# Identity matmuls ahead of the first scores, head 8's scores in other banks, and channel weights behind the v groups

## The chip, the cores and the metric

The kernel runs on one core of a Trainium2 chip. The metric is the device time of one execution in microseconds (us). Its engines are TensorE (PE in the profile, with PEld for its weight loads), VectorE (DVE), ScalarE (ACT), GpSimd (POOL) and SyncE (SP), which issues the DMA transfers. Each engine works through its own queue in order, and the queues meet in semaphores only.

## The reference

Three blocks follow each other, for a batch of 4, 8 heads, 576 positions and a head width of 64. Attention is masked by blocks of 64: query i sees key j where i // 64 >= j // 64.

```python
scores = scale * q @ k.T                      # per batch and head, masked by blocks of 64
attn = softmax(scores);  x = attn @ v         # heads side by side: x is (4, 576, 512)

h = relu(x @ w_in)                            # w_in 512 x 1024
u, v = h[..., :512], h[..., 512:]
v_n = (v - mean(v)) / sqrt(var(v) + 1e-6)
v_s = einsum('ts,bsd->btd', w_spatial, v_n) + b_spatial
y = (u * v_s) @ w_out                         # w_out 512 x 512

xn = (y - mean(y)) / sqrt(var(y) + 1e-6) * g_ln
out = y + relu(xn @ w_ch1) @ w_ch2            # w_ch1 512 x 2048, w_ch2 2048 x 512
```

## The kernel before

All of it is written out by hand, one instruction stream for each engine, with semaphores between them.

**Attention** takes 32 heads n = 0 to 31, eight to a batch. A head's queries are five tiles of up to 128 rows. Their order is 3, 0, 2, 1, 4 (`TILES`); the first three are the "first" tiles, the last two the "second" ones. For each, TensorE makes the scores in PSUM (L951) and adds a mask (L955), VectorE takes the row maximum (L759), ScalarE the exponential with its row sum (L564), VectorE inverts the sums (L767, L772), GpSimd multiplies them in (L476), TensorE transposes the result (L999), VectorE (L778) and ScalarE (L575, L576, L579) copy it out of PSUM, and TensorE multiplies by v (`attend`, L1013, L1018). The scale of q is put on by GpSimd (`scale_q`, L470). A head has four steps. On TensorE, step 0 of head n holds the first scores of head n+1, attend of head n-1 and the first transposes of head n; step 2 holds the second scores of head n+1 and the second transposes of head n.

**PSUM** has eight banks. First scores use banks 0 and 1. Second scores use two banks, given by `second_banks`: 2 and 3 for heads 0 to 7, and 1 and 2 from head 8 on, because banks 3 and 4 then belong to the mixer. With banks 1 and 2, second scores wait for the first exponentials of their own head (`score_second`), and the next head's first scores for all five (`score_first`).

**The mixer** (second block) of a batch is 26 groups of matmuls: 5 "v", 8 "u", 8 "s" and 5 "w" groups, numbered so that U0 = 5, S0 = 13 and W0 = 21. Groups of batch b are woven into the heads of batch b+1, some three to a head; the first one stands behind step 2 of head 8. They use banks 3 and 4 in turn, and each waits until the bank's last user was read (`bank_free`). A product is three FP32R matmuls of high and low parts (L1032, L1033, L1034). A v tile is copied out with a relu by ScalarE (L625), its mean and variance are made by VectorE (L812, L814, L816), the power -0.5 by GpSimd (L487), then VectorE normalises (L833), ScalarE makes the high part (L607) and VectorE the low part (L802); there are two buffers, so the copy of tile i waits for the low part of tile i-2. A u group is read by ScalarE (L629).

**The last mixer** (batch 3) has no heads beside it, and in its place the channel weights are prepared: 16 "units" of a column block of w_ch1 and a row block of w_ch2. A unit is loaded by SP, scaled with g_ln by GpSimd (`scale_unit`, L529), split in high parts by ScalarE (`split_unit`, L686, L687) and low parts by VectorE (L877, L879). `UNIT_AFTER` gives for the first ten units the group g at which GpSimd scales; ScalarE splits at g+1, VectorE at g+2, and SP then loads the unit four further on. GpSimd waits for nothing in u groups, so it runs ahead of the other engines there.

**The third block** takes six chunks of 384 rows with all 16 units (L1032 to L1034 again, L722, L925). The change leaves it as it is.

Of the kernel before, what the change touches and what calls it, by code (L numbers as in the profile page):

```python
# [27 lines left out]
P = 128  # L28
# [6 lines left out]
def transformer_block(nc, qk, vN, w_in, wsT, w_out, gT, w_ch1, w_ch2, out):  # L35
    B, H, D, S = qk.shape[0], qk.shape[1], qk.shape[2] // 2, qk.shape[3] // 2
# [5 lines left out]
    NT = -(-S // P)  # L42
# [18 lines left out]
    with ExitStack() as ctx:  # L61
        def sb(name, shape, dt=F32):
            return ctx.enter_context(nc.sbuf_tensor(name, shape, dt))

        def sem(name):
            return ctx.enter_context(nc.semaphore(name))
# [72 lines left out]
        ident = sb("ident", [P, P])  # L139
# [16 lines left out]
        psum = ctx.enter_context(nc.psum_tensor("psum", [P, 8, 512], F32))  # L156
        m_bank = psum[:, 3:5, :]
        o_bank = psum[:, 5, :]
        t_bank = psum[:, 6:8, :]
# [10 lines left out]
        ident_set = sem("ident_set")  # L170
# [3 lines left out]
        exped = sem("exped")  # L174
# [47 lines left out]
        U0, S0, W0 = NV, NV + NU, NV + NU + NS  # L222
# [3 lines left out]
        def kind_of(g):  # L226
            return ("v", g) if g < U0 else ("u", g - U0) if g < S0 else ("s", g - S0) if g < W0 else ("w", g - W0)
# [28 lines left out]
        AT = [TILES.index(t) for t in range(NT)]  # L256
        MADE = {3: 1, 0: 3, 2: 3, 1: 4, 4: 5}
        FIRST = 3

        def second_banks(n):  # L260
            return psum[:, 2:4, :] if n < H else psum[:, 1:3, :]

        def score_of(n, t):
            if t == 0:
                return psum[:, 1, KEYS[2]:KEYS[2] + KEYS[0]]
            if t == 2:
                return psum[:, 1, 0:KEYS[2]]
            if t == 3:
                return psum[:, 0, 0:KEYS[3]]
            if t == 1:  # L270
                return second_banks(n)[:, :, HALF:HALF + P]
            return second_banks(n)[0:LAST, :, 0:HALF]
# [28 lines left out]
        def bank_free(eng, b, g):  # L301

            if b == 0 and g < 2:
                if g == 0:
                    eng.wait_ge(exped, NT * H)
                return
            b, g = (b, g - 2) if g >= 2 else (b - 1, g - 2 + GROUPS)
            kind, i = kind_of(g)
            if kind == "s":
                eng.wait_ge(gate_raw, NS * b + i + 1)  # L310
            else:
                eng.wait_ge(copied, NCOPY * b + (g if g < S0 else g - NS) + 1)
# [27 lines left out]


        UNITS_EARLY = 10
        UNIT_AFTER = [1, 3, 5, S0 - 1, S0 + 1, S0 + 3, S0 + 5, W0 - 1, W0, W0 + 1]
        assert len(UNIT_AFTER) == UNITS_EARLY and UNIT_AFTER[-1] + 2 < GROUPS
        AFTER_U, AFTER_S, AFTER_W = 3, 7, 13
        assert UNITS + 2048 * AFTER_U <= MIXER and UNITS + 2048 * AFTER_S <= VN_END - 2 * NT * FFH
# [2 lines left out]
        def unit_at(g, lag):  # L349
            return [f for f, after in enumerate(UNIT_AFTER) if after + lag == g]  # L350

# [110 lines left out]
        def _(pool):  # L462
# [10 lines left out]
            def normalise(n, t):  # L473
                r, c = ROWS[t], slice(P_AT[t], P_AT[t] + KEYS[t])
                pool.wait_ge(inverted, 2 * n + (1 if AT[t] < FIRST else 2))
                pool.tensor_scalar(probs[0:r, n % 2, c], probs[0:r, n % 2, c], row_inv[0:r, n % 2, AT[t]:AT[t] + 1], 1.0,  # L476
                                   ALU.mult, ALU.mult).then_inc(normed, 1)
# [28 lines left out]
            pool.wait_ge(consts_set, 2)  # L506
            for t in TILES[:FIRST]:
                normalise(0, t)
            for n in range(HEADS):
                for step in range(STEPS):  # L510
                    if step == 0:
                        for t in TILES[FIRST:]:
                            normalise(n, t)
                        if n + 2 < HEADS:
                            scale_q(n + 2)
                    elif step == 1 and n + 1 < HEADS:
                        for t in TILES[:FIRST]:
                            normalise(n + 1, t)
# [34 lines left out]
        def _(act):  # L553
            def exp_tile(n, t):
                r, k, s = ROWS[t], KEYS[t], n % 2
                act.wait_ge(maxed, NT * n + PEAKS[t])
                if n >= 2:
                    act.wait_ge(t_made, NT * (n - 2) + AT[t] + 1)
                if n >= 2 and AT[t] == 0:
                    act.wait_ge(inverted, 2 * (n - 1))  # L560
                dst = probs[0:r, s, P_AT[t]:P_AT[t] + k]
                if t in TILES[FIRST:]:
                    dst = dst.rearrange("p (a n) -> p a n", a=2)
                act.activation(dst, score_of(n, t), ACT.Exp, bias=neg_max[0:r, s, AT[t]:AT[t] + 1],  # L564
                               accum_out=row_sum[0:r, s, AT[t]:AT[t] + 1]).then_inc(exped, 1)
# [74 lines left out]
            for n in range(HEADS):  # L640
                for step in range(STEPS):
# [5 lines left out]
                    if step == 0:  # L647
                        if n + 1 < HEADS:
                            for t in TILES[:FIRST]:
                                exp_tile(n + 1, t)  # L650
# [297 lines left out]
        def _(pe):  # L948
            def score(n, dst, half, rows, keys):

                return pe.matmul(dst, qk_raw[half, n % QS, 0, rows], qk_raw[half, n % QS, 1, keys],  # L951
                                 start=True, stop=True)

            def mask(dst, half):
                return pe.matmul(dst, row_pick[half, :], row_mask[half, :], start=False, stop=True,  # L955
                                 skip_group_check=True)
# [3 lines left out]
            def rows_of(t):  # L960
                return slice(P * t, P * t + ROWS[t])

            def score_first(n):

                pe.wait_ge(q_scaled, n + 1)
                if 1 <= n <= H:
                    pe.wait_ge(exped, NT * (n - 1) + FIRST)
                elif n > H:
                    pe.wait_ge(exped, NT * n)
                score(n, score_of(n, 3), LOW, rows_of(3), slice(0, KEYS[3]))  # L970
                score(n, score_of(n, 2), HIGH, rows_of(2), slice(0, KEYS[2]))
                mask(score_of(n, 2)[:, KEYS[2] - BLOCK:KEYS[2]], HIGH)
                score(n, score_of(n, 0), HIGH, rows_of(0), slice(0, KEYS[0]))
                mask(score_of(n, 0)[:, KEYS[0] - BLOCK:KEYS[0]], HIGH).then_inc(scored, 1)
                mask(score_of(n, 3)[:, KEYS[3] - BLOCK:KEYS[3]], LOW).then_inc(scored, 1)

            def score_second(n):

                if n >= H:
                    pe.wait_ge(exped, NT * n + FIRST)  # L980
                elif n >= 1:
                    pe.wait_ge(exped, NT * n)
                for half, part in enumerate((LOW, HIGH)):
                    score(n, score_of(n, 4)[:, half, :], part, rows_of(4), slice(HALF * half, HALF * (half + 1)))
                for half, part in enumerate((LOW, HIGH)):
                    last = score(n, score_of(n, 1)[:, half, :], part, rows_of(1), slice(P * half, P * (half + 1)))
                    if half == 1:
                        last = mask(score_of(n, 1)[:, half, P - BLOCK:P], part)
                    last.then_inc(scored, 1)
# [46 lines left out]
            def mixer(b, g):  # L1036
                kind, i = kind_of(g)
                bank_free(pe, b, g)
                bank = m_bank[:, (GROUPS * b + g) % 2, :]
                d, h = i // 2, slice(HALF * (i % 2), HALF * (i % 2 + 1))  # L1040
# [34 lines left out]
                                     w_out_lo[:, k, :], k == 0, k == KF - 1)  # L1075
                last.then_inc(grouped, 1)

            pe.wait_ge(consts_set, 12)
            score_first(0)
            score_second(0)  # L1080
            pe.wait_ge(ident_set, 2)
            for n in range(HEADS):
                for step in range(STEPS):
                    if step == 0:
                        if n + 1 < HEADS:
                            score_first(n + 1)
                        if n >= 1:
                            attend(n - 1)
                        for t in TILES[:FIRST]:
                            transpose_tile(n, t)  # L1090
                    elif step == 2:
                        if n + 1 < HEADS:
                            score_second(n + 1)
                        for t in TILES[FIRST:]:
                            transpose_tile(n, t)
                    for b, g in groups_at(n, step):
                        mixer(b, g)
# [83 lines left out]
```

## Time and profile before

| | |
|---|---|
| runs of the kernel | 844.64 us median of 3 (844.43 to 844.78) |
| the profiled execution | 845.24 us |
| its span, first to last instruction | 843.5 us |
| TensorE busy | 826.8 us, 98% |
| VectorE, ScalarE, GpSimd busy | 347.9, 291.9, 200.9 us |
| mean granted TensorE clock | 0.996 |

The page gives busy time by engine and cuts the span in 40 equal slices of 21.1 us, each digit a busy share or a granted clock in tenths, 9 for 90% or more. In a timeline a row is a run of like instructions: start, length, engine, line, operation, the tiles out and in with the shape, the count, and in brackets how long the engine idled before and which instruction released it. The length of a row with a count is from the first start to the last end. An FP32 matmul that is no transpose shows as two instructions in the records. Shapes such as 64*128 are the rows and columns of TensorE's array that are used. Times of the profiled execution are compared with its own total, not with the median.

### The profile page before, as it was taken

The numbers are of one execution on the slowest core, as the hardware profiler recorded it, in microseconds if no ns is written. First come the engines' busy times: TensorE is split into PE (matmuls) and PEld (weight loads), VectorE is DVE, ScalarE is ACT, GpSimd is POOL, SyncE is SP. The second block draws the span as 40 slices with busy tenths as digits, with TensorE's granted clock in tenths as the row PEclk, the third lists the DMA queues.
The fourth block names the chain that finished last, engine by engine and source line by source line (L and its number), as shares of the span: only waits on it lengthen the run. The fifth ranks groups of instructions, "written<-read, shape, count | busy, mean of one in ns | idle before, by whom it ended". The sixth has DMA issues, their size and how long they took to land.

```text
span 843.5 us, 13442 instructions
## 1 busy us (share of the span) xinstructions
PE 826.8 (98%) x5064; PEld 705.0 (84%) x5064; DVE 347.9 (41%) x774; ACT 291.9 (35%) x784; POOL 200.9 (24%) x289
## 2 busy tenths in 40 slices
PE   7989999999999999998999999999999999999998
PEld 4757888778887788877989999989999999999997
DVE  5876645466454665426573331321312313122111
ACT  5875664445554555424452111111111111111110
POOL 4875546323353234402631000000000000000000
PEclk9989999999999999999999999999999999999999
DMA  6451322221222220035251011003003003002001
GB/s 218 163 183 45 114 84 71 92 64 46 69 72 92 63 71 16 1 117 190 81 187 51 1 44 69 1 1 111 0 0 112 0 0 112 0 0 72 3 1 37
DMA packets 37681, 56.02 MB, mean 66 GB/s; under 512 B 2749, under 2 KB 20157, under 8 KB 37630
## 3 DMA queue, kind: packets, MB, share of 16 engines
q1 hardware_dynamic: 37630, 55.34, 19.7%
q8 instruction: 32, 0.52, 0.2%
q14 instruction: 19, 0.16, 0.1%
HBM read 45.90 MB, written 9.44 MB: 66 GB/s over the span
## 4 chain that ended last, share of the span: by engine, by line
PE 93%; issue 3%; DVE 2%; ACT 1%; POOL 1%; DMA 0%; ACTq 0%; POOLq 0%; DVEq 0%
PE psum L1032 24%; PE psum L1034 23%; PE psum L1033 23%; PE psum L951 8%; PE psum L999 7%; PE psum L1013 3%; PE psum L1018 2%; PE psum L1105 1%; DVE vn_r L802 1%; ACT probs L564 1%; DMA qk_raw<-qk 0%; PE psum L955 0%; DVE y_res L938 0%; DVE neg_max L759 0%; ACT units_r L686 0%
## 5 line engine op out<-in xcount | busy, mean ns | idle before, releaser
L925 DVE SCALAR_TENSOR_TENSOR h_r<-psum,h_r 128x384 fp32r<-128x384 f32 x96 | 53.5, 557 | 286.6 <-ACT h_r L722 286.6
L722 ACT ACTIVATE h_r<-psum 128x384 fp32r<-128x384 f32 x96 | 47.2, 491 | 340.6 <-PE psum L1034 340.6
L1032 PE MATMUL psum<-xn_r,units_r 128*128 128x384 f32 x384 | 129.6, 337 | 0.0
L1034 PE MATMUL psum<-xn_r,units_r 128*128 128x384 f32 x384 | 129.4, 337 | 0.0
L1033 PE MATMUL psum<-xn_r,units_r 128*128 128x384 f32 x384 | 128.9, 336 | 0.0
L476 POOL TENSOR_SCALAR probs<-probs,row_inv 128x512 f32<-128x512 f32 (+4 forms) x160 | 95.8, 612 | 125.3 <-DVE row_inv L772 125.3
L1034 PE MATMUL psum<-units_r,h_r 128*128 128x512 f32 x288 | 113.7, 395 | 0.0
L1033 PE MATMUL psum<-units_r,h_r 128*128 128x512 f32 x288 | 113.5, 394 | 0.0
L1032 PE MATMUL psum<-units_r,h_r 128*128 128x512 f32 x288 | 111.9, 389 | 0.0
L759 DVE TENSOR_REDUCE neg_max<-psum 128x1 f32<-128x512 f32 (+4 forms) x160 | 77.6, 535 | 78.1 <-PE psum L955 77.9
L564 ACT ACTIVATE probs<-psum,neg_max 128x512 f32<-128x512 f32 (+4 forms) x160 | 88.9, 563 | 45.9 <-DVE neg_max L759 45.7
L951 PE MATMUL psum<-qk_raw 64*128 64x128 f32 (+3 forms) x448 | 79.9, 445 | 8.5 <-POOL qk_raw L470 5.1
L1032 PEld LDWEIGHTS psum<-xn_r,units_r 128*128 128x128 f32 x384 | 72.2, 188 | 3.6
L1033 PEld LDWEIGHTS psum<-xn_r,units_r 128*128 128x128 f32 x384 | 72.1, 188 | 3.4
L534 POOL TENSOR_TENSOR c_rstd<-c_mean_var,neg_half 128x3 f32<-128x3 f32 x6 | 5.1, 851 | 291.0 <-DVE c_mean_var L893 291.0
L951 PEld LDWEIGHTS psum<-qk_raw 64*128 64x128 f32 (+1 forms) x448 | 37.2, 177 | 43.8 <-issue 41.5
L1034 PEld LDWEIGHTS psum<-xn_r,units_r 128*128 128x128 f32 x384 | 72.0, 188 | 0.0
L999 PE MATMUL psum<-ident,probs 128*128 128x128 f32 (+2 forms) x480 | 64.7, 270 | 0.6 <-DVE pt L778 0.6
L1034 PEld LDWEIGHTS psum<-units_r,h_r 128*128 128x128 f32 x288 | 54.0, 187 | 11.5
L1033 PEld LDWEIGHTS psum<-units_r,h_r 128*128 128x128 f32 x288 | 54.0, 188 | 9.4
L1032 PEld LDWEIGHTS psum<-units_r,h_r 128*128 128x128 f32 x288 | 54.1, 188 | 9.0
L999 PEld LDWEIGHTS psum<-ident,probs 128*128 128x128 f32 (+2 forms) x480 | 46.6, 140 | 11.2 <-issue 5.3
(101 smaller groups left out, 1459.8 us busy)
## 6 DMA issues: line engine op xcount, KB each, us to landing
qk_raw<-qk SPq DMA_DIRECT2D x32, 576.0 KB, 3.9
unit_raw<-w_ch SPq DMA_DIRECT2D x32, 256.0 KB, 3.7
y_norm<-y_scratch SPq DMA_DIRECT2D x6, 768.0 KB, 5.8
y_res<-y_scratch SPq DMA_DIRECT2D x6, 768.0 KB, 4.6
out<-y_res SPq DMA_DIRECT2D x18, 256.0 KB, 2.1
v_raw<-vN SPq DMA_DIRECT2D x16, 256.0 KB, 2.8
y_scratch<-mix_buf SPq DMA_DIRECT2D x16, 256.0 KB, 2.0
w_raw<-w_in SPq DMA_DIRECT2D x8, 256.0 KB, 4.7
```

The lines of the kernel that those rows point to most:

```text
L476: pool.tensor_scalar(probs[0:r, n % 2, c], probs[0:r, n % 2, c], row_inv[0:r, n % 2, AT[t]:AT[t] + 1], 1.0, ALU.mult, ALU.mult).then_inc(n ...
L564: act.activation(dst, score_of(n, t), ACT.Exp, bias=neg_max[0:r, s, AT[t]:AT[t] + 1], accum_out=row_sum[0:r, s, AT[t]:AT[t] + 1]).then_inc ...
L722: act.activation(h_hi[:, f % HR, :], h_bank[:, f % 2, 0:CHUNK], ACT.Relu).then_inc(h_hi_done, 1)
L759: dve.tensor_reduce(neg_max[0:r, s, AT[t]:AT[t] + 1], score_of(n, t), mybir.AxisListType.XY if t in TILES[FIRST:] else AX_X, ALU.max, nega ...
L925: dve.scalar_tensor_tensor(h_lo[:, f % HR, :], h_bank[:, f % 2, 0:CHUNK], 0.0, h_hi[:, f % HR, :].bitcast(F32), ALU.max, ALU.subtract).the ...
L951: return pe.matmul(dst, qk_raw[half, n % QS, 0, rows], qk_raw[half, n % QS, 1, keys], start=True, stop=True)
L999: last = pe.transpose(t_bank[0:k, bank, at + r * j:at + r * (j + 1)], probs[0:r, n % 2, c:c + k], ident[0:r, 0:r])
L1013: return pe.matmul(o_bank[0:D, P * j:SPLIT_Q], v_raw[:, s, j, cols], pt[:, PT_STEP * j + P * j:PT_STEP * j + SPLIT_Q], start=(j == 0), sto ...
L1018: return pe.matmul(o_bank[D:P, q - SPLIT_Q:S - SPLIT_Q], v_raw[:, s, j, cols], pt[:, PT_STEP * j + q:PT_STEP * j + S], start=(j == 0), sto ...
L1032: pe.matmul(dst, a_hi, b_hi, start=start, stop=False)
L1033: pe.matmul(dst, a_hi, b_lo, start=False, stop=False)
L1034: return pe.matmul(dst, a_lo, b_hi, start=False, stop=stop)
```

## The change

Three edits, which share no lines.

First, eight matmuls of the identity by itself are put ahead of the first scores. They wait for the identity, a wait that stood behind the first scores, and write to bank 6, which the transposes overwrite later.

Second, head 8 keeps banks 2 and 3 for its second scores: `n < H` becomes `n <= H`, the two waits of `score_first` and `score_second` move by one head, and the first mixer group, which uses bank 3, waits for the exponentials of head 8 instead of head 7.

Third, units 0, 1 and 2 are taken at groups 6, 8 and 10 (u groups) instead of 1, 3 and 5 (v groups).

```diff
+        WARM_UP = 8
 
         def second_banks(n):
-            return psum[:, 2:4, :] if n < H else psum[:, 1:3, :]
+            return psum[:, 2:4, :] if n <= H else psum[:, 1:3, :]
...
             if b == 0 and g < 2:
                 if g == 0:
-                    eng.wait_ge(exped, NT * H)
+                    eng.wait_ge(exped, NT * (H + 1))
                 return
...
-        UNIT_AFTER = [1, 3, 5, S0 - 1, S0 + 1, S0 + 3, S0 + 5, W0 - 1, W0, W0 + 1]
+        UNIT_AFTER = [U0 + 1, U0 + 3, U0 + 5, S0 - 1, S0 + 1, S0 + 3, S0 + 5, W0 - 1, W0, W0 + 1]
...
                 pe.wait_ge(q_scaled, n + 1)
-                if 1 <= n <= H:
+                if 1 <= n <= H + 1:
                     pe.wait_ge(exped, NT * (n - 1) + FIRST)
-                elif n > H:
+                elif n > H + 1:
                     pe.wait_ge(exped, NT * n)
...
             def score_second(n):
 
-                if n >= H:
+                if n > H:
                     pe.wait_ge(exped, NT * n + FIRST)
                 elif n >= 1:
                     pe.wait_ge(exped, NT * n)
...
+            pe.wait_ge(ident_set, 2)
+            for _ in range(WARM_UP):
+                pe.matmul(t_bank[:, 0, 0:P], ident[:, :], ident[:, :], start=True, stop=True)
             pe.wait_ge(consts_set, 12)
             score_first(0)
             score_second(0)
-            pe.wait_ge(ident_set, 2)
```

TensorE's queue begins, in the kernel before, with the first score matmuls (psum<-qk_raw) and their masks:

```order
L951 MATMUL psum<-qk_raw 128x512 [waits q_scaled,consts_set]
L951 MATMUL psum<-qk_raw 128x384
L955 MATMUL psum<-row_mask,row_pick 128x64
L951 MATMUL psum<-qk_raw 128x128
L955 MATMUL psum<-row_mask,row_pick 128x64 x2
```

and in the changed kernel, whose lines are numbered one to three higher, with the identity:

```order
L1081 MATMUL psum<-ident 128x128 [waits ident_set]
L1081 MATMUL psum<-ident 128x128 x7
L952 MATMUL psum<-qk_raw 128x512 [waits q_scaled,consts_set]
L952 MATMUL psum<-qk_raw 128x384
L956 MATMUL psum<-row_mask,row_pick 128x64
```

Eight matmuls stand ahead of the first scores, and nothing else in the queue has moved. The second edit moves no instruction; it changes banks and waits.

ScalarE's queue in the last mixer, before: v tiles are copied to mix_buf and their high parts made in vn_r, u groups go to u_buf, and units_r are the units' high parts.

```order
L625 ACTIVATE mix_buf<-psum 128x512 x2
L607 ACTIVATE vn_r<-mix_buf 128x512
L625 ACTIVATE mix_buf<-psum 128x512
L686 ACTIVATE units_r<-unit_raw 128x512
L687 ACTIVATE units_r<-unit_raw 128x512
L607 ACTIVATE vn_r<-mix_buf 128x512
L625 ACTIVATE mix_buf<-psum 128x512
L607 ACTIVATE vn_r<-mix_buf 128x512
L625 ACTIVATE mix_buf<-psum 64x512
L686 ACTIVATE units_r<-unit_raw 128x512
L687 ACTIVATE units_r<-unit_raw 128x512
L629 ACTIVATE u_buf<-psum 128x288
```

The same place in the changed kernel:

```order
L626 ACTIVATE mix_buf<-psum 128x512
L608 ACTIVATE vn_r<-mix_buf 128x512
L626 ACTIVATE mix_buf<-psum 128x512
L608 ACTIVATE vn_r<-mix_buf 128x512
L626 ACTIVATE mix_buf<-psum 64x512
L630 ACTIVATE u_buf<-psum 128x288
L608 ACTIVATE vn_r<-mix_buf 128x512
L630 ACTIVATE u_buf<-psum 128x288
L608 ACTIVATE vn_r<-mix_buf 64x512
L630 ACTIVATE u_buf<-psum 128x288
L687 ACTIVATE units_r<-unit_raw 128x512
L688 ACTIVATE units_r<-unit_raw 128x512
```

The first unit now stands behind the last v tile and the third u group.

GpSimd's queue in the last mixer, before, with the powers of the v tiles (rstd) and the scalings of units (unit_raw):

```order
L487 TENSOR_TENSOR rstd<-mean_var,neg_half 128x1 x2
L529 TENSOR_TENSOR unit_raw<-unit_raw,g_cols 128x512
L487 TENSOR_TENSOR rstd<-mean_var,neg_half 128x1 x2
L529 TENSOR_TENSOR unit_raw<-unit_raw,g_cols 128x512
L487 TENSOR_TENSOR rstd<-mean_var,neg_half 64x1
L529 TENSOR_TENSOR unit_raw<-unit_raw,g_cols 128x512 x2
L496 TENSOR_TENSOR x_r<-mix_buf,x_r 128x288 x2
```

and in the changed kernel:

```order
L488 TENSOR_TENSOR rstd<-mean_var,neg_half 128x1 x4
L488 TENSOR_TENSOR rstd<-mean_var,neg_half 64x1
L530 TENSOR_TENSOR unit_raw<-unit_raw,g_cols 128x512 x4
L497 TENSOR_TENSOR x_r<-mix_buf,x_r 128x288 x2
```

The four scalings of units 0 to 3 now stand together behind the five powers.

## Rows read from the trace of the kernel before

**Rows 1.** the page: TensorE busy, and granted clock in 40 slices

```profile
PE 826.8 (98%) x5064; PEld 705.0 (84%) x5064; DVE 347.9 (41%) x774; ACT 291.9 (35%) x784; POOL 200.9 (24%) x289
...
PEclk9989999999999999999999999999999999999999
```

**Rows 2.** timeline, first head: start us, us, engine line op, count [idle]

```profile
1.18 0.29 POOL L465 TENSOR_SCALAR_AFFINE_SELECT ident<-ident 128x128 f32<-128x128 f32 x1 [0.25 <-POOL ident L463]
...
4.29 0.67 POOL L470 TENSOR_SCALAR qk_raw<-qk_raw 128x576 f32<-128x576 f32 x1 [2.82 <-DMA qk_raw<-qk]
...
5.11 2.04 PE L951 MATMUL psum<-qk_raw 64*128 64x512 f32 x4 [5.11 <-POOL qk_raw L470]
...
10.08 2.04 PE L951 MATMUL psum<-qk_raw 64*128 64x512 f32 x4 [0.69 <-ACT probs L564]
...
12.36 1.97 PE L999 MATMUL psum<-ident,probs 128*128 128x128 f32 x8
...
12.44 0.19 ACT L564 ACTIVATION_READ_ACCUMULATOR probs<-psum,neg_max 64x1 f32 x1
...
13.22 0.69 ACT L564 ACTIVATE probs<-psum,neg_max 128x512 f32<-128x512 f32 x1 [0.59 <-DVE neg_max L759]
...
18.86 1.10 PE L999 MATMUL psum<-ident,probs 128*128 128x128 f32 x8
```

**Rows 3.** windows: length, busy us (count) by engine, PEclk, DMA

```profile
5.10:7.40 2.30, 2.29 (x11) 1.25 (x11) 0.00 (x0) 0.00 (x0) 0.67 (x1) 1.00 1.07 370
...
58.70:58.80 0.10, 0.00 (x0) 0.00 (x0) 0.00 (x0) 0.10 (x2) 0.10 (x1) 0.84 0.00 0
...
65.50:65.60 0.10, 0.10 (x2) 0.10 (x1) 0.10 (x1) 0.00 (x0) 0.00 (x0) 0.53 0.59 169
```

**Rows 4.** timeline of heads 6 to 9, TensorE, ScalarE and VectorE

```profile
47.85 1.09 PE L999 MATMUL psum<-ident,probs 128*128 128x128 f32 x8
...
52.33 0.20 ACT L564 ACTIVATION_READ_ACCUMULATOR probs<-psum,neg_max 64x1 f32 x1
...
53.32 1.09 PE L999 MATMUL psum<-ident,probs 128*128 128x128 f32 x8
...
55.25 1.12 PE L951 MATMUL psum<-qk_raw 64*64 64x288 f32 x8 [0.84 <-ACT probs L564]
...
56.46 1.08 DVE L759 TENSOR_REDUCE neg_max<-psum 128x1 f32<-128x256 f32 x2
...
59.05 2.04 PE L951 MATMUL psum<-qk_raw 64*128 64x512 f32 x4 [1.84 <-ACT probs L564]
...
64.28 1.71 PE L999 MATMUL psum<-ident,probs 128*128 128x128 f32 x8
...
67.82 0.50 PE L1032 MATMUL psum<-w_in_r,x_r 128*128 128x512 f32 x1
```

**Rows 5.** timeline of the last mixer's v and u groups

```profile
376.83 0.60 ACT L625 ACTIVATE mix_buf<-psum 128x512 f32<-128x512 f32 x1 [2.12 <-PE psum L1034]
...
387.63 0.59 ACT L625 ACTIVATE mix_buf<-psum 64x512 f32<-64x512 f32 x1 [3.35 <-DVE vn_r L802]
...
388.28 0.40 PE L1032 MATMUL psum<-x_r,w_in_r 128*128 128x288 f32 x1 [1.71 <-ACT mix_buf L625]
...
389.93 2.03 POOL L529 TENSOR_TENSOR unit_raw<-unit_raw,g_cols 128x512 f32<-128x512 f32 x2
...
390.11 2.40 DVE L802 TENSOR_TENSOR vn_r<-mix_buf,vn_r 128x512 fp32r<-128x512 f32 x1 [0.78 <-ACT vn_r L607]
...
395.02 0.40 PE L1032 MATMUL psum<-x_r,w_in_r 128*128 128x288 f32 x1 [1.70 <-ACT u_buf L629]
...
398.50 0.41 ACT L629 ACTIVATE u_buf<-psum 128x288 f32<-128x288 f32 x1 [1.19 <-PE psum L1034]
```

**Rows 6.** timeline, one VectorE subtract between GpSimd operations

```profile
150.04 1.89 DVE L794 TENSOR_TENSOR x_r<-x_acc,x_r 128x576 fp32r<-128x576 f32 x1
...
150.50 0.80 POOL L496 TENSOR_TENSOR gate_r<-mix_buf,gate_r 128x288 fp32r<-128x288 f32 x1
```
## The prediction

> **What bounds the kernel now.** I first read the page. TensorE is busy 826.8 of 843.5 us, and the granted clock is full in all but two early slices [rows 1]. So time can fall only where TensorE idles, 16.7 us in all, or where it runs at half rate. Next I read TensorE's timeline for idle time. The change touches three places: 5.11 us before the first score matmul [rows 2]; 0.84 and 1.84 us around head 8, the last part of attention without mixer work [rows 4]; 1.71 and 1.70 us in the last mixer's u groups [rows 5]. From 67.82 the first mixer group gives TensorE other work beside attention. Last I read the clock. It is granted at half (1.2 GHz of 2.4) from about 58.77 to 65.60: 0.84 over the tenth that ends at 58.80, 0.53 over the tenth that ends at 65.60 [rows 3]. TensorE had been idle in the 1.84 us wait when it fell. At the start the clock reads 1.00 [rows 3], but the durations contradict it: eight transposes take 1.97 us at 12.36 and 1.10 at 18.86, and the first scores 2.04, as those at 59.05 inside the half-rate stretch [rows 2, 4]. I take TensorE at 1.2 GHz there until the transposes at 12.36 are over.
>
> The sum is made against the profiled execution's 845.24 us (span 843.5, 1.74 around it), 0.60 above the median of 844.64; I take the 0.60 off at the end.
>
> **The banks of head 8.** Its second scores (tiles 1 and 4) go to banks 2 and 3, so they no longer wait for head 8's first exponentials, and head 9's first scores wait for these alone instead of all five. Nothing is added. Head 7's first transposes end at 53.32 + 1.09 = 54.41, its exponentials at 52.53 [rows 4], so the second scores start at once instead of at 55.25: 0.84 saved. They take 1.1 us, the seven transposes behind them 0.9 (eight take 1.09), and head 9's first scores start at 56.4, not at 59.05. What is late next: attend waits for a copy behind VectorE's maxima, which still end near 57.5 (56.46 + 1.08), so at 57.9: 0.3 us of idle. Then head 9's second scores: they wait for its first exponentials, which ScalarE starts after head 8's second ones, near 58.7, and ends near 60.4, when TensorE comes free too; I charge 0.2. The first mixer group waits for head 8's exponentials, over before 59.05 as it is [rows 4]. A head at full rate has 5.47 us between first transposes (47.85 to 53.32), this one 10.96 (53.32 to 64.28) [rows 4]. The excess of 5.49 is 2.68 of idle and 2.81 of work at half rate. **Term: -5.3 us**; ends -5.5 (the whole excess) and -2.4 (idle less 0.3, the half rate stays).
>
> **The channel weights.** Units 0 to 2 leave the v groups: three GpSimd scalings, six ScalarE copies and six VectorE subtracts go behind them. Six loads of units 4 to 6 go with them, each issued when its slot is free; SP's queue holds no store between, and their use comes after the u groups as before. Before, v tile 4's copy waited 3.35 us for a VectorE subtract and held TensorE 1.71, and a second wait for a u copy held it 1.70 [rows 5]. Without the units the v tiles come at TensorE's own pace of 2.72 us (the 2.12 idle and 0.60 busy of ScalarE before 376.83 show it) [rows 5]. VectorE then has one tile's statistics, normalising and subtract per 2.72 us, less work than that, so tile 4's copy should come three tiles after 376.83, at 385.0, and end at 385.6. From the end of that copy (387.63 + 0.59) to the end of the tile's power on GpSimd (389.93) it took 1.7 before [rows 5]: 387.3.
>
> There is a new cost. GpSimd then has four scalings in a row, until 387.3 + 4 x 1.02 = 391.4, since the u groups hold it nowhere. The trace shows what that does to VectorE's subtract: begun at 390.11 beside two scalings (389.93 to 391.96), it took 2.40 and ended 0.55 after them [rows 5], so it ran only when GpSimd had finished. Elsewhere one waited through the boundary between two GpSimd operations (150.04, a second one at 150.50) and ended at 151.93, 0.63 after the second [rows 6]. In the changed kernel tile 3's subtract starts near 387.6, then tile 4's normalising, then ScalarE's copy of tile 4, and only behind that ScalarE reads the third u bank. TensorE needs it when u groups 0 to 3 are over: 385.0 + 4 x 1.60 = 391.4 (1.60 is 1.19 idle and 0.41 busy of ScalarE's u reads [rows 5]). If VectorE is shut out until 391.4, then 0.55 each for the subtract and the normalising (as long as the subtract ran alone), 0.6 for the copy and 0.4 for the read end at 393.5, and TensorE idles 2.1. If it gets in between, the idle is between 0 and that. I take 1.2. **Term: -3.41 + 1.2 = -2.2 us**, ends -3.4 and -1.3. The rest of the move is hidden: tile 4's subtract must be done when the s groups start, near 397.8, and the u phase leaves ScalarE 1.19 us idle of each 1.60, in which the unit copies, every second group, nearly fit.
>
> The Trainium skill (SBUF — State Buffer, section "SBUF: two separate sides") says that the port pair of VectorE and GpSimd is an exclusive lock: whoever starts first has it for the whole instruction and the other fully blocks. Read so, the subtract would get in after one scaling, and the term would be near -3.4. The row at 390.11 agrees with the blocking, but shows the waiter passed over once more.
>
> **The warm-up.** The identity is ready at 1.18 + 0.29 = 1.47, so eight matmuls start near 1.5. They are FP32, and I take two passes each, since the two first score matmuls show as x4 [rows 2]. A pass like a transpose at half rate takes (1.97 - 0.2) / 8 = 0.22 us [rows 2]: 16 x 0.22 = 3.5, over at 5.05. The first scores started at 5.11 after the scaling that ends at 4.96, so they lose 0 to 0.4. The transposes no longer wait for the identity, long set. What can be gained is full rate before 14.3. If TensorE runs full from 7.5 on, head 1's first scores and head 0's transposes take half their 2.2 and 1.97, 1.9 us less on TensorE, but then ScalarE is late: its exponentials of head 0 end at 12.63 and head 1's began at 13.22 [rows 2], so 0.6 comes through, some 1.6 if the first scores run full as well. But TensorE already waits 0.69 us for the first exponentials before 10.08, at half rate [rows 2]; with its second scores done at full rate, 0.9 us sooner, it waits 1.5, and the clock fell at 58.77 in an idle of 1.84. If it falls there, head 0 and 1 run slower than now, up to half of 3 us. **Term: -0.2 us**, ends -1.6 and +1.5.
>
> The Trainium skill (TensorE: Matmul & The Clock Gate, section "What's actually happening") says that the throttled state is the default and activity releases it. The durations at 5.11 agree, the granted clock shown there does not; by that reading alone the warm-up would gain, by the 1.00 of the row nothing.
>
> **Sum.** 845.24 - 5.3 - 2.2 - 0.2 = 837.5; less 0.6 it is 836.9, and I say 837.0.
>
> **The rivals.**
> - The lock costs nothing: VectorE gets in between GpSimd's scalings, or its work is early enough. For it: the pass-over was seen with two scalings, not four. Against: the row at 390.11. Time 837.0 - 1.2 = 835.8.
> - The warm-up pays in full: half rate ends before the first scores. For it: TensorE then works without a break from 1.5. Against: the wait before 10.08. Time 837.0 - 1.4 = 835.6.
> - The half rate around head 9 stays: the idle that is left (0.3 + 0.2), in a stretch of FP32 work, is enough. For it: the clock fell in such a stretch. Against: the slices of heads 1 to 7, the same work, read full or nearly so [rows 1]. Time 837.0 + 2.9 = 839.9.
> - The change doesn't do what it says: ScalarE or VectorE sets the pace of head 8 as of the heads before, and the first mixer group starts no earlier than 67.8. Against: that pace is 5.47 us, not 10.96 [rows 4]. With -1.3 of the last mixer alone it is 843.3; within 0.2% only if that fails too.
> - Slower: the clock as one mechanism. Each fall costs 6.83 us of half rate, in dense mixer work 3.4. If the waits that move (head 0's before 10, head 9's, the 2.1 us in the u groups) each draw a fall, the terms become +1.5, +0.4 (3.4 of new half rate instead of 2.81, most of the idle kept) and -1.3 + 3.4: together +4.0, 848.6. It decides from three falls on; two leave it faster. Against: 1.71 and 1.70 us of idle in the u groups drew none [rows 1, 5].
>
> **How the numbers follow.** Forecast 0.46; lock free 0.17; warm-up in full 0.12; half rate stays 0.17; it doesn't do what it says 0.05; slower 0.03. The likeliest is 837.0. The range 834.2 to 840.2 holds the first four with their ends, leaving out the last two and combined ends. A measurement of this kernel tells 0.2%, 1.7 us, from no change. The first four cases are all faster by more than that: 0.92; same 0.05; slower 0.03.
>
> **What would show it.** The granted clock full from 50 to 70, no idle of TensorE over 0.5 us before the first mixer group, and 5.3 us less between head 7's first transposes and that group, prove the first term; a half-rate stretch there breaks it. In the last mixer, no wait of a v copy for VectorE, one wait of TensorE at the fifth u group of 0 to 2.1 us, and a VectorE subtract stretched by GpSimd prove the second. For the warm-up: 16 passes of 0.22 us, the first scores no later than 5.5, and head 0's transposes near 1.1 us or near 2. A first mixer group after 64 would make the forecast wrong.

## The result, and the profile after

The changed kernel takes 838.67 us (median of 4 runs, 837.04 to 839.52), the kernel before 844.71 (4 runs). The ratio is 0.9924, 95% interval 0.991 to 0.9937: some 6 us faster. A second series of five runs gave 0.9919 (0.9906 to 0.9931). The profiled execution took 839.52 us, the slowest of the four, its span 837.7.

The page of the kernel after, for [rows 1]: TensorE is as busy as before in a shorter span, and the slice with 8 in the clock is gone.

```profile
PE 827.1 (99%) x5080; PEld 706.9 (84%) x5080; DVE 348.1 (42%) x774; ACT 292.6 (35%) x784; POOL 201.7 (24%) x289
...
PEclk9999999999999999999999999999999999999999
```

TensorE in the first head, after, for [rows 2]:

```profile
1.53 3.78 PE L1081 MATMUL psum<-ident 128*128 128x128 f32 x16 [1.53 <-POOL ident L466]
5.62 1.77 PE L952 MATMUL psum<-qk_raw 64*128 64x512 f32 x4 [0.31 <-POOL qk_raw L471]
...
10.19 1.84 PE L952 MATMUL psum<-qk_raw 64*128 64x512 f32 x4 [1.55 <-ACT probs L565]
...
12.30 1.81 PE L1000 MATMUL psum<-ident,probs 128*128 128x128 f32 x8
...
18.81 1.09 PE L1000 MATMUL psum<-ident,probs 128*128 128x128 f32 x8
```

The sixteen passes take 3.78 us, and the first scores start 0.5 us later than before. TensorE then waits 1.55 us for the first exponentials, and the clock falls to half. The two windows show it, with the granted clock third from the end of each row:

```profile
7.00:10.40 3.40, 1.85 (x18) 1.07 (x17) 1.64 (x6) 1.69 (x6) 0.00 (x0) 1.00 1.04 379
10.41:13.80 3.39, 3.39 (x16) 2.34 (x15) 2.38 (x7) 1.91 (x6) 1.61 (x3) 0.50 0.76 257
```

So head 1's first transposes start at 18.81 instead of 18.86, and nothing is won here. Heads 7 to 9, for [rows 4]:

```profile
53.28 1.09 PE L1000 MATMUL psum<-ident,probs 128*128 128x128 f32 x8
54.31 1.12 PE L952 MATMUL psum<-qk_raw 64*64 64x288 f32 x8
...
57.74 0.51 PE L1014 MATMUL psum<-pt,v_raw 128*64 128x392 f32 x1 [0.41 <-issue]
...
59.26 1.09 PE L1000 MATMUL psum<-ident,probs 128*128 128x128 f32 x8
...
62.18 0.50 PE L1033 MATMUL psum<-w_in_r,x_r 128*128 128x512 f32 x1
```

The waits of 0.84 and 1.84 us are gone and 0.41 is left, for which the profile names no releaser ("issue"); the last copy that attend needs, behind VectorE's maxima, ends at 57.64. There is no half rate, and the first mixer group starts 5.64 us sooner. The last mixer, for [rows 5], first GpSimd and VectorE, then ScalarE, then TensorE:

```profile
381.67 4.03 POOL L530 TENSOR_TENSOR unit_raw<-unit_raw,g_cols 128x512 f32<-128x512 f32 x4
```

```profile
381.91 4.34 DVE L803 TENSOR_TENSOR vn_r<-mix_buf,vn_r 128x512 fp32r<-128x512 f32 x1 [0.84 <-ACT vn_r L608]
```

```profile
371.17 0.60 ACT L626 ACTIVATE mix_buf<-psum 128x512 f32<-128x512 f32 x1 [2.12 <-PE psum L1035]
...
386.74 0.63 ACT L608 ACTIVATE vn_r<-mix_buf 64x512 fp32r<-64x512 f32 x1 [3.79 <-DVE mix_buf L834]
```

```profile
387.72 0.41 PE L1033 MATMUL psum<-x_r,w_in_r 128*128 128x288 f32 x1 [2.03 <-ACT u_buf L630]
...
395.74 0.29 PE L1033 MATMUL psum<-ws_r,vn_r 128*128 128x288 f32 x1
```

VectorE's subtract starts 0.24 us after the first scaling has begun and ends 0.55 us after the fourth has ended. ScalarE makes tile 4's high part (vn_r) only when VectorE has subtracted and normalised, so the third u bank is read late, and TensorE idles 2.03 us. From 389.3 to 392.7 the clock is then at half once more:

```profile
389.20:389.30 0.10, 0.10 (x3) 0.10 (x3) 0.10 (x1) 0.00 (x0) 0.00 (x0) 0.95 0.00 0
...
389.30:392.70 3.40, 3.40 (x17) 3.40 (x16) 2.03 (x4) 1.50 (x4) 0.00 (x0) 0.50 0.30 84
...
392.70:392.80 0.10, 0.10 (x2) 0.10 (x2) 0.00 (x0) 0.10 (x1) 0.00 (x0) 0.98 0.47 102
```

In the kernel before, the first s matmul ran at 401.48:

```profile
401.48 0.29 PE L1032 MATMUL psum<-ws_r,vn_r 128*128 128x288 f32 x1
```

From the second v copy to the first s matmul it took 401.48 - 376.83 = 24.65 us before and 395.74 - 371.17 = 24.57 after. In this profile nearly the whole gain is that of the banks.

### The profile page after: what moved, and what is told of

It is laid out like the page before. It is cut to its first block, busy times and chain, and to the rows that moved or that the text cites. A ratio compares the mean times of both kernels' runs of the same rounds, so it can differ in the third digit from the quotient of the medians.

```text
span 837.7 us, 13474 instructions
## 1 busy us (share of the span) xinstructions
PE 827.1 (99%) x5080; PEld 706.9 (84%) x5080; DVE 348.1 (42%) x774; ACT 292.6 (35%) x784; POOL 201.7 (24%) x289
## 4 chain that ended last, share of the span: by engine, by line
PE 97%; DVE 1%; DMA 0%; issue 0%; ACT 0%; POOL 0%; ACTq 0%; DVEq 0%
PE psum L1033 25%; PE psum L1035 25%; PE psum L1034 25%; PE psum L952 8%; PE psum L1000 7%; PE psum L1014 3%; PE psum L1019 3%; PE psum L1108 1%; DVE vn_r L803 1%; DMA qk_raw<-qk 0%; PE psum L956 0%; DVE y_res L939 0%; DVE neg_max L760 0%; ACT probs L565 0%; DVE row_sum L768 0%
## 5 line engine op out<-in xcount | busy, mean ns | idle before, releaser
L952 PE MATMUL psum<-qk_raw 64*128 64x128 f32 (+3 forms) x448 | 77.4, 433 | 1.9 <-ACT probs L565 1.6
```

## The experiments

Four places of TensorE's work cut each profile in comparable stretches. "First mixer" is from head 1's first transposes to the first mixer group, "last mixer" from the second v copy to the first s matmul (us, profiled execution):

| kernel | head 1's first transposes at | first mixer | last mixer | span |
|---|---|---|---|---|
| before | 18.86 | 48.96 | 24.65 | 843.5 |
| changed | 18.81 | 43.37 | 24.57 | 837.7 |
| warm_only | 17.02 | 48.86 | 24.67 | 841.5 |
| banks_only | 18.91 | 43.38 | 24.67 | 837.9 |
| weights_only | 18.88 | 47.44 | 23.01 | 840.3 |
| all_three | 18.00 | 43.38 | 23.03 | 835.4 |
| gated | 16.96 | 43.36 | 20.86 | 832.1 |
| gated_b | 17.19 | 43.35 | 20.86 | 832.3 |
| gated_no_warm_b | 19.14 | 43.36 | 20.86 | 834.3 |
| gated_warm_filled | 17.42 | 43.35 | 20.87 | 832.6 |
| idle_filled | 17.91 | 45.92 | 24.66 | 839.4 |
| warm_filled | 16.81 | 43.36 | 24.53 | 835.7 |
| u_wait_filled_b | 16.86 | 43.37 | 23.01 | 834.2 |

The kernel before itself spreads from 841.0 to 845.6 us over all series, so the small ratios need their intervals.

The record also has the mean granted clock of every run, profiled or not. The profiles show what it stands for: at 0.999 and 1.000 they have no stretch of half rate, at 0.998 one of 3.4 us (weights_only, warm_filled), at 0.995 and 0.996 two of them (changed) or one of 6.8 (before, warm_only). I read 0.997 as one and 0.994 as three, which no profile shows. Half rate behind TensorE's last matmul, where it costs nothing, lowers the figure by up to 0.001, and the half rate at the very start isn't in it, since the clock reads 1.00 there. Sorted so, the times are (us, number of runs in brackets, stretches counted in pieces of 3.4 us):

| kernel | none | one | two | three |
|---|---|---|---|---|
| before, series of warm_only | 841.18 to 841.37 (3) | 842.81 to 844.74 (7) | 843.62 to 845.45 (13) | |
| changed, both series | 835.98, 837.18 | 837.04 to 838.12 (5) | 839.23, 839.52 | |
| warm_only | | 842.85, 842.93 | 842.72 to 843.76 (7) | 844.65, 844.79 |
| banks_only | 838.63 to 840.49 (5) | | | |
| weights_only | 839.63 | 841.26 to 842.94 (3) | 842.29 to 843.38 (5) | 845.1 to 845.33 (3) |
| idle_filled | 841.13 to 842.4 (5) | | | |
| gated and gated_b | 834.04 to 834.21 (4) | 835.47 to 835.61 (6) | | |
| gated_no_warm_b | 834.92 to 836.2 (6) | | | |
| warm_filled | 836.21 to 837.08 (3) | 837.46 | | |
| gated_warm_filled | 834.63 to 835.78 (4) | | | |
| u_wait_filled_b | 836.06 to 837.1 (5) | 837.55 | | |

**The warm-up alone.**

```diff
+        WARM_UP = 8
...
+            pe.wait_ge(ident_set, 2)
+            for _ in range(WARM_UP):
+                pe.matmul(t_bank[:, 0, 0:P], ident[:, :], ident[:, :], start=True, stop=True)
             pe.wait_ge(consts_set, 12)
             score_first(0)
             score_second(0)
-            pe.wait_ge(ident_set, 2)
```

> The kernel before with the eight identity matmuls alone. Theory: the warm-up ends half rate early (near 7.0), the wait of 1.5 us for the first exponentials draws a fall of the clock near 10.4, and what is won is lost again: first transposes of head 1 start at 18.8 us (18.86 before), the total is 844.6, ratio 1.000 within 0.001. Rival: the warm-up brings part of the 5.8 us that the three edits bring together; then 843.5 or less.

Measured 843.3 us (median of 11 runs) against 843.89, ratio 0.9995 (0.9986 to 1.0004): no difference on the mean. Yet this profile had no fall near 10.4, and was 1.84 us ahead at head 1. So the warm-up can pay up to 1.8 us. In the table its runs have 2.0 pieces of half rate on average and those of before 1.4 (22 / 11 and 33 / 23), none of its runs is free of it, and two have three. This fits a fall at the start in some executions, as the theory has it for all; no profile of this kernel shows one.

```profile
17.02 1.09 PE L1000 MATMUL psum<-ident,probs 128*128 128x128 f32 x8
```

**The banks alone.**

```diff
-            return psum[:, 2:4, :] if n < H else psum[:, 1:3, :]
+            return psum[:, 2:4, :] if n <= H else psum[:, 1:3, :]
...
-                    eng.wait_ge(exped, NT * H)
+                    eng.wait_ge(exped, NT * (H + 1))
...
-                if 1 <= n <= H:
+                if 1 <= n <= H + 1:
                     pe.wait_ge(exped, NT * (n - 1) + FIRST)
-                elif n > H:
+                elif n > H + 1:
...
-                if n >= H:
+                if n > H:
                     pe.wait_ge(exped, NT * n + FIRST)
```

> The kernel before with head 8's second scores in banks 2 and 3 alone. Theory: the two waits of 0.84 and 1.84 us and the half-rate stretch from 58.8 to 65.6 go, the first mixer group starts at 62.2 instead of 67.8, and the last mixer waits as before: 844.7 - 5.6 = 839.1, ratio 0.9934. Rival: the half rate was not drawn by the waits and stays, 842.0. Rival: the warm-up is needed for it, anything from 840 to 844.

Measured 839.69 us (5 runs), ratio 0.9948 (0.9935 to 0.9961), so 3.3 to 5.5 us, 4.4 in the middle. The stretch to the first mixer group is 5.58 us shorter, as forecast, and needs no warm-up; no run shows half rate. The mean gains less because before's half rate is not always 6.8 us long. An estimate from the table: (13 x 6.83 + 7 x 3.4) / 23 = 4.9 us of it in a run of before, which loses 1.0 us less than 6.83 do. That is most of the 1.2 between 5.58 and 4.4; the rest is open.

```profile
62.29 0.50 PE L1032 MATMUL psum<-w_in_r,x_r 128*128 128x512 f32 x1
```

**The channel weights alone.**

```diff
-        UNIT_AFTER = [1, 3, 5, S0 - 1, S0 + 1, S0 + 3, S0 + 5, W0 - 1, W0, W0 + 1]
+        UNIT_AFTER = [U0 + 1, U0 + 3, U0 + 5, S0 - 1, S0 + 1, S0 + 3, S0 + 5, W0 - 1, W0, W0 + 1]
```

> The kernel before with units 0 to 2 taken in the u groups alone. Theory: the 1.71 and 1.70 us waits go, VectorE's subtract of v tile 3 is shut out for 4 us by GpSimd's four scalings, TensorE waits 2.0 us at the fifth u group, a gain of 1.4 us; where the clock falls behind that wait, 1.3 us of it are lost again. So 843.3 with no fall, 844.6 with one, and the runs lie between. Rival: the edit's gain is 3.4 and only the other edits take it away, 841.3.

Measured 842.82 us (12 runs, 839.63 to 845.33), ratio 0.9992 (0.9978 to 1.0006): no difference that the runs can tell, and far from the 3.4 of the rival. The wait is the 2.0 us of the changed kernel, here without a fall, and the last mixer is 1.64 us shorter. The one run without any half rate, 839.63, is 1.6 us below before's three; three runs have one piece of half rate more than any run of before.

```profile
391.84 0.40 PE L1032 MATMUL psum<-x_r,w_in_r 128*128 128x288 f32 x1 [2.02 <-ACT u_buf L629]
```

In the same profile the half rate at head 9, which this edit does not touch, was over after 3.4 us, half as long as in [rows 3]:

```profile
58.80:62.30 3.50, 3.20 (x14) 2.03 (x16) 0.78 (x2) 0.21 (x3) 0.29 (x1) 0.52 0.60 196
62.40:66.00 3.60, 3.60 (x36) 2.64 (x33) 2.47 (x8) 2.90 (x10) 2.42 (x4) 1.00 0.39 127
```

That is worth 1.5 us (48.96 - 47.44), and such differences make much of the spread of the kernel before, by the table above.

**All three, again.** The changed kernel, unedited.

> The changed kernel once more, on the same chip as the three parts. Theory: the parts add up, with -0 (warm-up), -5.6 (banks) and -0.1 to -1.4 (weights): 837.7 to 839.1, runs spread by 1 to 2.5 us because the clock falls in the last mixer in some and not in others; the profile here shows 1 or 0 half-rate stretches between 380 and 400 us. Rival: the spread comes from the start, then the start of the first mixer group differs by over 1 us from the 62.18 of the first profile.

Measured 837.44 us (5 runs), 0.9919 (0.9906 to 0.9931), span of the profile 835.4. This profile has no fall anywhere: 18.00 at head 1 and 23.03 in the last mixer. Of the 2.3 us between it and the first profile, 0.8 are at the start (18.81 against 18.00) and 1.5 in the last mixer. So the theory holds the larger part of the spread. The start holds the rest, though with 0.8 us it stays below the 1 us that the rival asked for (61.38 against 62.18).

**A gate before the scalings.** GpSimd waits for the last low part of v:

```diff
                 for f in unit_at(g, 0):
+                    if f == 0:
+                        pool.wait_ge(vn_lo_done, NT * B)
                     scale_unit(f)
```

> The changed kernel, but GpSimd begins the four scalings only when VectorE has made the low part of the last v tile. Theory (port held by GpSimd): VectorE's subtract of v tile 3 takes 0.68 us instead of 4.34, the third u bank is read on time, the wait of 2.03 us before the fifth u group is gone or under 0.5, and from the second v copy to the first s matmul it takes 21.2 us instead of 23.0 to 24.6; 1.8 to 3.3 us less than the changed kernel. Rival: the subtract is slow because of DMA traffic or of ScalarE, which the gate leaves as they are; then it still takes over 2 us and the time is that of the changed kernel.

Measured 834.83 us (4 runs), ratio 0.9886 (0.9871 to 0.9901). VectorE and GpSimd, in the gated kernel:

```profile
380.05 0.69 DVE L805 TENSOR_TENSOR vn_r<-mix_buf,vn_r 128x512 fp32r<-128x512 f32 x1 [0.84 <-ACT vn_r L610]
```

```profile
382.65 4.49 POOL L530 TENSOR_TENSOR unit_raw<-unit_raw,g_cols 128x512 f32<-128x512 f32 x4 [2.83 <-DVE vn_r L805]
```

The same subtract takes 0.69 instead of 4.34 us. TensorE has no wait left in the last mixer, which takes 20.86 us, a little less than the 21.2 expected. This is the shut-out shown by its removal. The rivals fall in the changed kernel itself: while its subtract stood for 4.34 us, ScalarE was busy for 0.41 us and no DMA ran.

```profile
381.90:386.30 4.40, 3.79 (x29) 3.55 (x27) 4.39 (x2) 0.41 (x1) 3.80 (x4) 1.00 0.00 0
```

Not every subtract is shut out until the end of a row. Behind the gate one of the unit subtracts (L880) begins inside the third of the four scalings:

```profile
384.98 1.26 DVE L880 TENSOR_TENSOR units_r<-unit_raw,units_r 128x512 fp32r<-128x512 f32 x1 [2.40 <-ACT units_r L690]
```

It is over at 386.24, while the row goes on to 387.14, and the fourth scaling takes 1.49 us where the first three took 1.04. So VectorE got in at the first boundary it met, and the same in all four gated profiles (1.26 or 1.27 us). In the five profiles with the weights edit and without the gate, the v subtract took 4.33 or 4.34 us each time. What decides between the two is open.

**Fillers in the wait before head 9,** in the kernel before:

```diff
+                        if n == H:
+                            for _ in range(7):
+                                pe.matmul(psum[:, 4, 0:P], ident[:, :], ident[:, :], start=True, stop=True)
                         if n + 1 < HEADS:
                             score_first(n + 1)
```

> The kernel before with seven more identity matmuls, to an unused bank, in TensorE's wait of 1.84 us ahead of head 9's first scores. Theory (an idle TensorE draws the fall): the first mixer group can start no earlier than the waits allow, but there is no half rate behind them, so it starts near 65.0 instead of 67.8; 1.5 to 2.8 us faster than before, and the rest of the 5.6 us of the banks edit is the idle itself. Rival: the fall comes from the kind of work (64-row FP32 scores); then half rate is granted again near 58.8 to 65.6 and the time is that of before or up to 0.3 us more.

Measured 841.25 us (5 runs), ratio 0.9965 (0.9951 to 0.9978). The matmuls fill the wait, the clock stays, and the stretch is 3.04 us shorter, though head 9's first scores wait for the same exponentials as before. (The group starts at 63.83 and not at 65.0 because this execution was 0.95 us sooner at head 1.)

```profile
56.21 1.83 PE L1087 MATMUL psum<-ident 128*128 128x128 f32 x14
...
63.83 0.50 PE L1032 MATMUL psum<-w_in_r,x_r 128*128 128x512 f32 x1
```

```profile
58.00:62.00 4.00, 3.92 (x38) 1.00 0.64 221
62.00:66.00 4.00, 4.00 (x25) 1.00 0.70 201
```

So of the 5.58 us of the banks edit, 3.04 are half rate drawn by the idle, 2.54 the idle itself. The kind of work was the same, so the rival falls, and not by one profile alone: none of the five runs has half rate by its mean clock (0.999 or 1.000), and all nine runs of before in this series have it (0.996 to 0.998).

**Fillers at the start.** The changed kernel with six more behind the second scores of head 0:

```diff
             score_second(0)
+            for _ in range(6):
+                pe.matmul(t_bank[:, 0, 0:P], ident[:, :], ident[:, :], start=True, stop=True)
```

> The changed kernel with six more identity matmuls behind head 0's second scores, where TensorE waits 1.55 us. Theory: no half rate from 10.4 on in any run, head 7's first transposes start at 51.5 to 52.5 in the profile, and the median is 0.5 to 1 us below that of the changed kernel (837.4 here). Rival: the fillers are too few or the fall is not drawn by that wait, and nothing changes beyond 0.3 us; or they delay head 1's first scores, up to 0.5 us more.

Measured 836.99 us (4 runs), 0.9905 (0.989 to 0.992), overlapping 0.9919. The profile has 16.81 at head 1 and 51.27 at head 7, just ahead of the 51.5 expected, so the start did its part. But a fall in the last mixer (24.53) took the gain back in that execution, so "no half rate from 10.4 on in any run" missed. On the mean the run is inconclusive.

**Gate and fillers.** Both edits in one kernel.

> The changed kernel with both: the gate before the four scalings and the six fillers behind head 0's second scores. Theory: the two gains add up, 837.4 - 2.2 - 0.7 = 834.5, ratio to before 0.989, and the runs spread by less than 1.5 us since no wait is left that draws a fall. Rival: one gain only, 835.2 to 836.7.

Measured 834.87 us (4 runs), 0.9887 (0.9872 to 0.9902), runs from 834.63 to 835.78: the same as the gate alone on the mean. None of its four runs has half rate, against two of the four of gated, but gated's two free runs are faster, 834.04 and 834.17. So the fillers may keep the clock and cost about as much; four runs don't settle it.

**The gate with and without the warm-up.** The gated kernel again, and with `WARM_UP = 0`.

> The gated kernel once more, beside itself without the warm-up. Theory: 0.9886 of before again, within 0.001, and no half-rate stretch between the start and the last chunk.

> The gated kernel without the eight identity matmuls. Theory: the clock rises at 8.7 to 14.6 us instead of 4.6 to 7.7, as in the kernels without warm-up so far, and head 1's first transposes start at 17.9 to 18.9 instead of 17.0 to 18.0; 0.5 to 1.5 us slower than the gated kernel. Rival: the warm-up is worth nothing on the mean, as its own run beside before said (0.9995), and the two are within 0.3 us.

Measured 835.47 and 835.48 us (6 runs each), ratios 0.9908 (0.9892 to 0.9924) and 0.991 (0.9894 to 0.9926) to a before of 843.73. The ratio missed the expected 0.9886, in part because this series' before had three runs of 841; the medians of the two series with the gate agree within 0.7 us. The profile without the warm-up has head 1's first transposes at 19.14, just outside the 17.9 to 18.9 expected, with it at 17.19. But the medians are equal, so the rival was right, and the table shows why. With the warm-up two of the six runs are free of half rate, at 834.09 and 834.21, and four have one piece, at 835.47 to 835.51; without it none has a piece, and they take 834.92 to 836.2. So the warm-up gains in some executions and draws a fall in others. This also breaks "no half-rate stretch between the start and the last chunk" of the expectation. No profile caught such a fall in a gated kernel; the only wait of that length that is left there is the 1.55 us for head 0's first exponentials.

**Fillers in the last mixer's wait,** in the changed kernel:

```diff
+                if g == U0 + 4:
+                    for _ in range(8):
+                        pe.matmul(t_bank[:, 1, 0:P], ident[:, :], ident[:, :], start=True, stop=True)
                 mixer(B - 1, g)
```

> The changed kernel with eight more identity matmuls in TensorE's wait of 2.03 us ahead of the fifth u group, to an unused bank. Theory: no half-rate stretch behind it in the profile or the mean, the time is the best of the changed kernel, 836.0 to 837.0 (0.9910 of before or less), and the 2.03 us are still lost. Rival: the fall near 389 had another cause; then a half-rate stretch of 3.4 us shows there in this kernel too, and the spread of the changed kernel (1.5 to 2.5 us) stays.

Measured 836.46 us (6 runs, 836.06 to 837.55), ratio 0.9926 (0.991 to 0.9942). The profile has no half rate there and 23.01 us in the last mixer, so the 2.03 us stay lost. The time is as expected, the ratio, by the same low before, is not. Five of the six runs are free of half rate, against two of nine of the changed kernel, and the sixth has one piece at a place unknown. This agrees with a fall drawn by the idle, and proves no more than that.

## Why the prediction came true, and where it did not

The time was inside the range, 1.7 us above the 837.0 forecast. Against the profiled execution, for which the terms were summed, it was 839.52 to 837.5: the channel weights came out 2.1 us too dear, and the banks 0.3 better.

- **The banks, -5.3 us.** The mechanism was right: -5.6 in the profiles, with the split in 2.7 idle and 2.8 half rate measured as 2.5 and 3.0. The remaining 0.3 us of idle before attend was 0.41; the 0.2 charged for head 9's second scores did not come. That the number came so close is partly luck. The excess of 5.49 less 0.3 and 0.2 is 4.99 and not 5.3, and the profiles have 10.96 - 5.98 = 4.98 between the first transposes of heads 7 and 9. What makes it 5.6 is half rate behind 64.28, which the sum left out: from those transposes to the first mixer group it took 67.82 - 64.28 = 3.54 us before and 62.18 - 59.26 = 2.92 after. On the mean of the runs the gain was 4.4 (3.3 to 5.5), because I took one execution's 6.83 us of half rate for every execution's. And [rows 1] has one slice below 9, not two; a 9 stands for 90% or more and can't show a full clock.
- **The channel weights, -2.2 us.** The step that failed is "I take 1.2" for TensorE's new wait. The mechanism was the predicted one, VectorE behind four scalings, but it was passed over at all three boundaries, so the wait was 2.03, the 2.1 of my upper bound. And the term allowed no fall of the clock there, since waits of 1.7 us had drawn none [rows 5]; only the slower rival had one, at 3.4 us, and the fall cost 1.5 (24.57 against 23.03). It came in two of the profiles with this wait (changed, warm_filled) and not in two (weights_only, all_three). The edit gave -1.6 without and -0.1 with it.
- **The warm-up, -0.2 us.** Right on the mean (0.9995). The passes took 0.24 us against 0.22, and the fall after the 1.5 us wait came in the first profile as described, but not in warm_only or all_three. Where it doesn't come, head 1 is up to 1.9 us ahead (16.96 in gated), more than the -1.6 of the upper end.
- **The lock.** What the prediction draws from the Trainium skill (SBUF — State Buffer, section "SBUF: two separate sides") agrees with the traces as far as the blocking goes. The reading that the waiter gets in after one instruction failed for the v subtract, 4.34 us behind four scalings of 1.03, and held for the unit subtract in the gated kernels, 1.26 us.

The rival of half rate that stays at head 9 is excluded by every profile with the banks edit; that of a fall at several places came in part, with two falls, and left the kernel faster as it said.

## What to carry to other kernels

An idle of TensorE of 1.5 to 2 us cost twice here: its own length and, in some executions, 3.4 or 6.8 us at half rate behind it, which is 1.5 to 3 us of time. Moving GpSimd work out of one engine's way can put it in a row in front of another: look at where the moved instructions now stand together, and gate them behind the VectorE work that others wait for. Here one wait instruction took 2.2 us from the last mixer where the clock did not fall (23.03 to 20.86) and 3.7 where it had (24.57), more than any other part after the banks. The kernels with the gate are the fastest found, 834.83 and 835.47 us in two series; with the fillers, or without the warm-up, they take as long (834.87, 835.48). And one profile is one execution: the mean granted clock of every run says whether it is a typical one.

## What the runs showed of the hardware

- A VectorE subtract with both inputs in SBUF can stand behind a whole row of GpSimd operations: 4.34 us behind four of 1.03, against 0.69 alone. Another got in at the next boundary (1.26 us, gated), so who comes first there is open.
- The same program is granted half rate differently from one execution to the next: the mean clock of before's 23 runs in one series is 0.996 in 13, 0.997 or 0.998 in 7 and 0.999 or 1.000 in 3. At head 9 the stretch was 6.83 us in the profile of before and 3.4 in that of weights_only, whose work up to there is the same.
- The clock fell behind idles of TensorE of 1.55, 1.84 and 2.03 us, each in some executions and not in others, and did not fall where matmuls of the identity filled the 1.84 us (five runs of five).
- The granted clock reads 1.00 at the start, though the identity passes take 3.78 / 16 = 0.24 us there and 1.83 / 14 = 0.13 us at full rate (idle_filled); only durations show the rate there.
